# Scores of the next tile between the state's part and D, one output group per tile, D in a bank of its own

## The chip, the cores and the metric

The kernel runs on one core of a Trainium2 chip. The time is the device time of one execution in microseconds (us). The kernel before takes 898.84 us, the median of 3 runs (898.82 to 900.29).

## What is computed

Three layers follow one another. Everything is fp32, and the matmuls of the layers split each operand into a high and a low part (three products for one).

```python
# linear attention with decay, B=4 H=8 S=768 D=64
state = gamma * state + outer(k[t], v[t]);  y[t] = scale * q[t] @ state
# x: (3072, 512).  Layer 1, d_ff 1024:
h = x @ w_in;  sm = exp(h - max(h)) / (sum + 1e-9);  solu = h * sm
x = layernorm(solu) * g_ln @ w_out
# Layer 2, d_ff 2048:
h = x @ w_in;  out = (h * cos(h)) @ w_out
```

## The kernel before

The first half of the kernel (up to about 380 us) runs attention and layer 1 over 24 tiles of 128 tokens, six per batch. The second half runs layer 2 and is not touched. A tile passes through stages that are spread over several steps, so in step n the engines work on tiles n down to n - 4. One list, `STEP`, gives the stages of a step in order, each with how many tiles it lies behind. Every engine runs the same list in order and skips the names that it has no code for. Nothing but semaphores ties the engines together. The first tiles have lists of their own (`pe_first`, `act_first`, `dve_first`, `pool_first`), and a tail of hand-written order ends the half.

The stages on TensorE (PE), with the line of each matmul:

- SC (L558): scores of a tile, 16 instructions with 64 rows each, pairs of heads side by side. They fill banks 0 and 1 of PSUM (`ps_p`).
- OS (L582): the part of the output that comes from the state, 8 instructions. Left out for the first tile of a batch.
- DL (L570): D, the tile's own contribution to the state, 16 instructions with 64 columns each. It writes `ps_d`, which lies over banks 0 and 1, so SC must wait until the state has been brought up to date, and DL until the scores have been read. Left out for the last tile of a batch.
- OP (L599): masked scores times v, 16 instructions. OS and OP add up in `ps_o`, two pairs of heads in bank 2 and two in bank 3, and `o_done` rises twice per tile.
- L1a, L1b (L318 to L321, the three products): layer 1's first matrix, 12 instructions of 512 columns for each half.
- T0, T1 (L636): transposes of the centred result. T1 waits for z_l of T0, T0 for VectorE's CEN.
- L2a, L2b: layer 1's second matrix, 24 instructions. YT (L671): transposes of its result.

VectorE (DVE) masks the scores (L1055, SC), takes the low parts of x (L1076, O0 and O1) and of z (L1129, T0 and T1), takes the row maximum (L1095, L1b), copies YT (L1141), multiplies h by exp (L1101, U), adds D to the state (L1070, ST), centres (L1115, CEN), and in between splits the second layer's weights into low parts (L1149, WE, and L1144, WD). ScalarE (ACT) makes the high parts (x_h L774, z_h L800), exp (L794), the square (L809), y (L805) and the high parts of the weights (L815, L818, both in WH at the end of a step, ahead of the next step's T0). GpSimd (POOL) scales q (L967) and k, decays the state (L980) and adds weights.

SyncE (SP) issues all DMAs. `swap_unit` stores what WD and WE made and loads the next weights; it waits for WE of the last unit before it stores that unit (L457) and loads the next one (L461), which ScalarE's L818 waits for. There is one such unit in tiles 0 to 4 of the last three batches and one in the first batch.

Of the kernel before, what the change touches and what calls it, by code (L numbers as in the profile page):

```python
# [26 lines left out]
F32 = mybir.dt.float32  # L27
# [3 lines left out]
B, H, S, D = 4, 8, 768, 64  # L31
PAIRS = H // 2
# [52 lines left out]

STEP = [("PK", 0), ("PV", 0), ("SG", 1), ("L1a", 2), ("SC", 1), ("T0", 3), ("L1b", 2), ("T1", 3),
        ("EX", 2), ("OS", 1), ("DL", 1), ("OP", 1), ("YT", 4), ("U", 2), ("O0", 1), ("O1", 1), ("ST", 1),
        ("WS", 0), ("WE", 1), ("L2a", 3), ("SQ", 2), ("L2b", 3), ("CEN", 2), ("VAR", 2),
        ("WH", 0), ("WD", 0)]
LAG = 4  # L90


def build(nc, qT, kT, kn, vn, consts, w1_in, w1_out, g_ln, w2_in, w2_out, y_scratch, w2_split,
          w2o_split, out):
    ctx = ExitStack()
    with ctx:
# [5 lines left out]
        ps_p = bank[:, 0:2, :].rearrange("p a (c t) -> p c a t", c=PAIRS)  # L102
        ps_o = bank[:, 2:4, 0:2 * C]

        ps_d = bank[:, 0:2, :].rearrange("p g (j n) -> p (g j) n", j=2)[:, :, 0:D]
        ps_h = bank[:, 4:6, :]
# [133 lines left out]
        def unit(b, n):  # L240
# [8 lines left out]
                    ("L1a0", 0), ("L1b0", 0), ("L1a1", 0), ("L1b1", 0), ("SC", 2), ("OS", 2),  # L249
                    ("DL", 2), ("OP", 2), ("L1a", 1), ("T0", 0), ("L1b", 1), ("T1", 0), ("LA", 0),  # L250
                    ("LB", 0), ("LC", 0), ("LD", 0)]
        act_first = [("O0", 0), ("O1", 0), ("W1H", 0), ("W1H", 1), ("O0", 1), ("O1", 1), ("W1H", 2),
                     ("W1H", 3), ("EX", 0), ("W1H", 4), ("O0", 2), ("SQ", 0), ("O1", 2), ("W1H", 5),
                     ("T0", 0), ("W1H", 6), ("W1H", 7), ("T1", 0), ("EX", 1), ("SQ", 1), ("LD", 0)]
        dve_first = [("QS", 0), ("ID", 0), ("SC0", 0), ("SC1", 0), ("O0", 0), ("ST", 0), ("O1", 0),
# [4 lines left out]
                     ("CEN", 1), ("VAR", 1)]  # L260
# [29 lines left out]
        def wait_state(eng, s, batch, tile):  # L290

            wait(eng, s, batch, tile // TILES * (TILES - 1) + min(tile % TILES, TILES - 2),
                 per_batch=TILES - 1)
# [31 lines left out]
        def rows(a):  # L325

            return slice(a * D, (a + 1) * D)
# [56 lines left out]
        def _(sp):  # L384
# [12 lines left out]
            def load_next(t, slot):  # L397


                sp.wait_ge(o_done, 2 * t)  # L400
                if isinstance(t, int) and t == 1:
                    sp.wait_ge(d_done, 1)
                load_kq(t + 2, slot)
                load_nv(t + 2, slot)
# [118 lines left out]
            load_y(0)  # L523
            sp.wait_ge(o_done, 2 * NT)
            load_split(0, 0)
# [19 lines left out]
        def _(pe):  # L545
            def step(name, t, b):
                par = t % 2
                if name == "SC":

                    wait(pe, q_sc, b, t)  # L550
                    if t % TILES > 0:
                        wait_state(pe, st_done, b, t - 1)
                    wait(pe, pm_done, b, t - 1, 2, 1)
# [8 lines left out]
                elif name == "DL" and t % TILES < TILES - 1:  # L562

                    wait(pe, n_sc, b, t)
                    wait(pe, pm_done, b, t, 2, 1)
                    for p in range(PAIRS):
# [7 lines left out]
                elif name == "OS" and t % TILES > 0:  # L574
# [4 lines left out]
                    wait(pe, q_sc, b, t)  # L579
                    wait(pe, xl_done, b, t - 1, 2, 1)  # L580
                    for p in range(PAIRS):
                        pe.matmul(ps_o[:, p // 2, p % 2 * C:(p % 2 + 1) * C],  # L582
                                  s_32[:, (t % TILES - 1) % 2, p, :, :].rearrange("p a n -> p (a n)"),
                                  raw[:, t % RAW, 0, p * C:(p + 1) * C],
                                  start=p % 2 == 0, stop=False)
                elif name == "OP":
# [3 lines left out]
                    else:  # L590
                        wait(pe, n_sc, b, t)
                    wait(pe, xl_done, b, t - 1, 2, 1)
                    for p in range(PAIRS):
                        if p % 2 == 0:
                            wait(pe, pm_done, b, t, 2, p // 2)
                        for a in range(2):
                            h = slice((2 * p + a) * D, (2 * p + a + 1) * D)
                            o = slice((p % 2 * 2 + a) * C, (p % 2 * 2 + a + 1) * C)
                            m = pe.matmul(ps_o[rows(a), p // 2, p % 2 * C:(p % 2 + 1) * C],  # L599
                                          raw[:, t % RAW, 3, h], p_m[:, p // 2, o],  # L600
                                          start=p % 2 == 0 and t % TILES == 0, stop=p % 2 == 1,
                                          tile_position=(0, a * D))
                        if p % 2 == 1:
                            m.then_inc(o_done, 1)
                elif name[:3] in ("L1a", "L1b"):
# [5 lines left out]
                    for k in ks:  # L611
                        if half == 0 and isinstance(b, int) and t == 0:
                            pe.wait_ge(w1_lo, k + 1)
                        if half == 0 and k % 2 == 0:
                            wait(pe, xl_done, b, t, 2, k // 2)
                        m = products(pe, ps_h[:, half, :], [
                            (x_h[:, par, k, :], x_l[:, par, k, :],
                             w1i_h[:, k, cols], w1i_l[:, k, cols])], k == 0, k == KD - 1)
# [146 lines left out]
        def _(act):  # L765
# [3 lines left out]
            def step(name, t, b):  # L769
                par = t % 2  # L770
                if name in ("O0", "O1"):
                    g = int(name == "O1")
                    wait(act, o_done, b, t, 2, g)
                    act.copy(x_h[:, par, 2 * g:2 * g + 2, :],  # L774
                             ps_o[:, g, :].rearrange("p (j t) -> p j t", j=2))\
                        .then_inc(xh_done, 1)
                elif name == "W1H":
# [50 lines left out]
            def y_hi(i, p):  # L828
                if p in (P1, P2, P3):
                    act.wait_ge(ld_y, i * 16 + 16)  # L830
                else:
                    block_wait(act, {P6: t2_done, P5: t1_done, P7: t3_done, P4: t4_done}[p],
                               i, 1, 0)
                if isinstance(i, int) and i == 0:
                    act.wait_ge(o_done, 2 * NT)
                else:
                    at(act, p_done[p], i, -1)
                act.copy(yc_h[:, p, :, :], operand[p]).then_inc(yh_done, 1)
# [119 lines left out]
        def _(pool):  # L958
            pool.memset(mhalf[:, :], -0.5).then_inc(setup, 1)

            def step(name, t, b):
# [12 lines left out]
                elif name == "SG" and 0 < t % TILES < TILES - 1:  # L974
                    c = t % TILES
                    wait_state(pool, st_done, b, t - 1)
                    wait(pool, o_done, b, t - 1, 2, 1)
                    new, old = [s_32[:, n % 2, :, :, :].rearrange("p c a n -> p c (a n)")
# [55 lines left out]
        def _(dve):  # L1034
# [4 lines left out]
            def step(name, t, b):  # L1039
# [5 lines left out]
                elif name == "QS":  # L1045
                    q = raw[:, t % RAW, 0, :]
                    loaded(dve, ld_kq, t, b)
                    dve.tensor_tensor(q, q, qsc, ALU.mult).then_inc(q_sc, 1)
                elif name in ("SC", "SC0", "SC1"):
                    if isinstance(b, int) and t == 0:  # L1050
                        dve.wait_ge(ld_mask, 16)
                    for g in [int(name[2])] if name[2:] else range(2):
                        wait(dve, qk_done, b, t)
                        wait(dve, o_done, b, t - 1, 2, g)
                        dve.tensor_tensor(two_pairs(p_m[:, g, :]), ps_p[:, 2 * g:2 * g + 2, :, :],  # L1055
                                          mask[:, 4 * g:4 * g + 4, :].rearrange(
                                              "p (j a) t -> p j a t", j=2),
                                          ALU.mult).then_inc(pm_done, 1)
                elif name == "ST" and c < TILES - 1:

                    wait_state(dve, d_done, b, t)
                    wait(dve, o_done, b, t - 1, 2, 1)
                    new = s_32[:, c % 2, :, :, :]
# [8 lines left out]
                    m.then_inc(st_done, 1)  # L1072
                elif name in ("O0", "O1"):
                    g = int(name == "O1")
                    wait(dve, xh_done, b, t, 2, g)
                    dve.tensor_tensor(x_l[:, par, 2 * g:2 * g + 2, :],  # L1076
                                      ps_o[:, g, :].rearrange("p (j t) -> p j t", j=2),
                                      x_h[:, par, 2 * g:2 * g + 2, :].bitcast(F32),
                                      ALU.subtract).then_inc(xl_done, 1)
# [261 lines left out]
```

## Time and profile before

| | |
|---|---|
| median of 3 runs | 898.84 us |
| profiled execution | 900.71 us |
| its span (first to last instruction) | 898.9 us |
| TensorE busy | 883.4 us (98%) |
| VectorE busy | 570.6 us (63%) |
| ScalarE busy | 439.3 us (49%) |
| GpSimd busy | 142.5 us (16%) |
| granted TensorE clock, mean | 1.000 |

A busy TensorE counts overlapping matmuls once. The pitch, from one instruction's start to the next one's, tells what an instruction costs. A matmul of 512 columns has a duration of 0.39 us and a pitch of 0.23 us.

### The profile page before, as it was taken

The numbers are of one execution on the slowest core, as the hardware profiler recorded it, in microseconds if no ns is written. First come the engines' busy times: TensorE is split into PE (matmuls) and PEld (weight loads), VectorE is DVE, ScalarE is ACT, GpSimd is POOL, SyncE is SP. The second block draws the span as 40 slices with busy tenths as digits, with TensorE's granted clock in tenths as the row PEclk, the third lists the DMA queues.
The fourth block names the chain that finished last, engine by engine and source line by source line (L and its number), as shares of the span: only waits on it lengthen the run. The fifth ranks groups of instructions, "written<-read, shape, count | busy, mean of one in ns | idle before, by whom it ended". The sixth has DMA issues, their size and how long they took to land.

```text
span 898.9 us, 14463 instructions
## 1 busy us (share of the span) xinstructions
PE 883.4 (98%) x5184; PEld 771.0 (86%) x5184; DVE 570.6 (63%) x872; ACT 439.3 (49%) x687; POOL 142.5 (16%) x187
## 2 busy tenths in 40 slices
PE   5899999999999999999999999999999999999998
PEld 4788888888888888889999999899999999999997
DVE  4956566566665666576665866566765658765654
ACT  3433344244333434366555755455655547554553
POOL 3242434225333342310000000000000000000000
PEclk9999999999999999999999999999999999999999
DMA  9534465636555463758954447444365444454401
GB/s 340 177 113 131 158 223 171 215 111 233 205 177 174 166 241 118 235 187 300 305 190 118 120 115 249 134 112 123 110 198 186 120 115 118 119 183 121 113 0 71
DMA packets 106662, 148.18 MB, mean 165 GB/s; under 512 B 7424, under 2 KB 77184, under 8 KB 106624
## 3 DMA queue, kind: packets, MB, share of 16 engines
q1 hardware_dynamic: 106624, 147.69, 51.3%
q8 instruction: 21, 0.34, 0.2%
q14 instruction: 17, 0.14, 0.0%
HBM read 112.01 MB, written 35.65 MB: 164 GB/s over the span
## 4 chain that ended last, share of the span: by engine, by line
PE 96%; DVE 2%; DMA 1%; issue 1%; SPq 0%; ACT 0%; DVEq 0%
PE bank L318 28%; PE bank L321 28%; PE bank L320 28%; PE bank L558 3%; PE bank L636 3%; PE bank L599 2%; PE bank L582 2%; PE bank L671 2%; PE bank L570 1%; DVE w1i_l L1084 1%; DMA raw<-kT 1%; DVE w1o_l L1089 0%; DVE nmax L1095 0%; DMA out<-o_a 0%; DVE s L1070 0%
## 5 line engine op out<-in xcount | busy, mean ns | idle before, releaser
L318 PE MATMUL bank<-yc_h,ring 128*128 128x384 f32 x448 | 151.5, 338 | 0.0
L320 PE MATMUL bank<-yc_l,ring 128*128 128x384 f32 x448 | 151.4, 338 | 0.0
L321 PE MATMUL bank<-yc_h,ring 128*128 128x384 f32 x448 | 150.9, 337 | 0.0
L1178 DVE SCALAR_TENSOR_TENSOR gg<-turns,c 128x768 f32<-128x768 int32 x64 | 61.0, 954 | 63.8 <-ACT turns L846 63.8
L852 ACT ACTIVATE gg<-gg 128x768 f32<-128x768 f32 x64 | 54.1, 846 | 80.2 <-DVE gg L1185 80.1
L846 ACT ACTIVATE turns<-c 128x768 int32<-128x768 f32 x64 | 54.2, 846 | 79.1 <-DVE c L1248 76.6
L318 PEld LDWEIGHTS bank<-yc_h,ring 128*128 128x128 f32 x448 | 84.1, 188 | 8.0 <-issue 0.5
L320 PEld LDWEIGHTS bank<-yc_l,ring 128*128 128x128 f32 x448 | 84.2, 188 | 7.2
L321 PEld LDWEIGHTS bank<-yc_h,ring 128*128 128x128 f32 x448 | 84.1, 188 | 0.0
L318 PE MATMUL bank<-w1i_h,x_h 128*128 128x512 f32 x192 | 77.5, 404 | 1.6 <-DVE w1i_l L1084 1.6
L318 PE MATMUL bank<-w1o_h,z_h 128*128 128x512 f32 x192 | 77.2, 402 | 1.1 <-DVE z_l L1129 1.1
L321 PE MATMUL bank<-w1o_h,z_l 128*128 128x512 f32 x192 | 75.2, 391 | 0.0
L321 PE MATMUL bank<-w1i_h,x_l 128*128 128x512 f32 x192 | 75.0, 391 | 0.0
L321 PE MATMUL bank<-w2o,glo_l 128*128 128x512 f32 x192 | 75.0, 391 | 0.0
L320 PE MATMUL bank<-w2o,glo_h 128*128 128x512 f32 x192 | 75.0, 391 | 0.0
L320 PE MATMUL bank<-w2o,ghi_h 128*128 128x512 f32 x192 | 74.9, 390 | 0.0
L800 ACT CAST z_h<-bank 128x512 fp32r<-128x512 f32 x48 | 28.2, 587 | 95.5 <-PE bank L636 95.5
L320 PE MATMUL bank<-w1i_l,x_h 128*128 128x512 f32 x192 | 74.8, 390 | 0.0
L321 PE MATMUL bank<-w2o,ghi_l 128*128 128x512 f32 x192 | 74.8, 390 | 0.0
L320 PE MATMUL bank<-w1o_l,z_h 128*128 128x512 f32 x192 | 74.7, 389 | 0.0
L318 PE MATMUL bank<-w2o,glo_h 128*128 128x512 f32 x192 | 74.6, 389 | 0.0
L318 PE MATMUL bank<-w2o,ghi_h 128*128 128x512 f32 x192 | 74.6, 388 | 0.0
(99 smaller groups left out, 1701.3 us busy)
## 6 DMA issues: line engine op xcount, KB each, us to landing
ring<-w_split SPq DMA_DIRECT2D x224, 256.0 KB, 2.8
w_split<-w_out SPq DMA_DIRECT2D x16, 896.0 KB, 6.3
w2o_split<-wo_out SPq DMA_DIRECT2D x16, 512.0 KB, 2.9
w2o<-w2o_split SPq DMA_DIRECT2D x8, 1024.0 KB, 7.7
raw<-qT SPq DMA_DIRECT2D x24, 256.0 KB, 4.4
raw<-kT SPq DMA_DIRECT2D x24, 256.0 KB, 3.5
raw<-kn SPq DMA_DIRECT2D x24, 256.0 KB, 4.5
raw<-vn SPq DMA_DIRECT2D x24, 256.0 KB, 5.1
```

Of the source, the lines that this page charges most:

```text
L318: eng.matmul(dst, ah, bh, start=first and i == 0, stop=False, skip_group_check=read_between)
L320: eng.matmul(dst, ah, bl, start=False, stop=False, skip_group_check=read_between)
L321: m = eng.matmul(dst, al, bh, start=False, stop=last_one and i == n - 1, skip_group_check=read_between)
L558: m = pe.matmul(ps_p[:, p, a, :], raw[rows(a), t % RAW, 1, cols], raw[rows(a), t % RAW, 0, cols], start=True, stop=True, tile_position=(a ...
L582: pe.matmul(ps_o[:, p // 2, p % 2 * C:(p % 2 + 1) * C], s_32[:, (t % TILES - 1) % 2, p, :, :].rearrange("p a n -> p (a n)"), raw[:, t % RA ...
L599: m = pe.matmul(ps_o[rows(a), p // 2, p % 2 * C:(p % 2 + 1) * C], raw[:, t % RAW, 3, h], p_m[:, p // 2, o], start=p % 2 == 0 and t % TILES ...
L636: m = pe.transpose(ps_t[:, k * 128:(k + 1) * 128], c_b[:, (4 * g + k) * 128:(4 * g + k + 1) * 128], ident[:, :])
L671: m = pe.transpose(ps_t[:, k * 128:(k + 1) * 128], y32[:, k * 128:(k + 1) * 128], ident[:, :])
L800: act.copy(z_h[:, 4 * g:4 * g + 4, :].rearrange("p k t -> p (k t)"), ps_t[:, :])\
L846: act.activation(turns[:, r, :], flat(c_32[:, r, :, :]), ACT.Copy, scale=INV_2PI)\
L852: act.activation(gg[:, r, :], gg[:, r, :], ACT.Sin, scale=0.5)\
L1178: dve.scalar_tensor_tensor(gg[:, r, :], turns[:, r, :], -TWO_PI_HI, flat(c_32[:, r, :, :]), ALU.mult, ALU.add)\
```

## The change

SC of tile n moves from its place after L1a of step n + 1 (where it was one tile behind) to step n, between OS and DL of tile n - 1. The masking on VectorE gets the name SM and stands between U and X. Output and D get one bank each (2 and 3), apart from the scores. The output is one accumulation group per tile: the first pair alone starts it, `o_done` rises once, and O0 and O1 become one operation X on ScalarE and one on VectorE. SC no longer waits for the state; DL waits for the previous state in place of p_m. L1a waits for all of x_l at once. In the opening SC of tile 3 comes before the first L2 products, and in the tail there is no SC left.

```diff
-STEP = [("PK", 0), ("PV", 0), ("SG", 1), ("L1a", 2), ("SC", 1), ("T0", 3), ("L1b", 2), ("T1", 3),
-        ("EX", 2), ("OS", 1), ("DL", 1), ("OP", 1), ("YT", 4), ("U", 2), ("O0", 1), ("O1", 1), ("ST", 1),
-        ("WS", 0), ("WE", 1), ("L2a", 3), ("SQ", 2), ("L2b", 3), ("CEN", 2), ("VAR", 2),
-        ("WH", 0), ("WD", 0)]
+STEP = [("PK", 0), ("PV", 0), ("SG", 1), ("L1a", 2), ("T0", 3), ("L1b", 2), ("T1", 3), ("EX", 2),
+        ("OS", 1), ("SC", 0), ("DL", 1), ("OP", 1), ("YT", 4), ("U", 2), ("SM", 0), ("X", 1),
+        ("ST", 1), ("WS", 0), ("WE", 1), ("L2a", 3), ("SQ", 2), ("L2b", 3), ("CEN", 2),
+        ("VAR", 2), ("WH", 0), ("WD", 0)]
...
-        ps_o = bank[:, 2:4, 0:2 * C]
-        ps_d = bank[:, 0:2, :].rearrange("p g (j n) -> p (g j) n", j=2)[:, :, 0:D]
+        ps_o = bank[:, 2, :].rearrange("p (c t) -> p c t", c=PAIRS)
+        ps_d = bank[:, 3, 0:PAIRS * D].rearrange("p (c n) -> p c n", c=PAIRS)
...
         pe_first = [("SC", 0), ("OP", 0), ("DL", 0), ("SC", 1), ("OS", 1), ("DL", 1), ("OP", 1),
                     ("L1a0", 0), ("L1b0", 0), ("L1a1", 0), ("L1b1", 0), ("SC", 2), ("OS", 2),
-                    ("DL", 2), ("OP", 2), ("L1a", 1), ("T0", 0), ("L1b", 1), ("T1", 0), ("LA", 0),
-                    ("LB", 0), ("LC", 0), ("LD", 0)]
+                    ("DL", 2), ("OP", 2), ("L1a", 1), ("T0", 0), ("L1b", 1), ("T1", 0), ("SC", 3),
+                    ("LA", 0), ("LB", 0), ("LC", 0), ("LD", 0)]
...
                 if name == "SC":
                     wait(pe, q_sc, b, t)
-                    if t % TILES > 0:
-                        wait_state(pe, st_done, b, t - 1)
                     wait(pe, pm_done, b, t - 1, 2, 1)
...
                 elif name == "DL" and t % TILES < TILES - 1:
                     wait(pe, n_sc, b, t)
-                    wait(pe, pm_done, b, t, 2, 1)
+                    wait_state(pe, st_done, b, t - 1)
...
-                            m = pe.matmul(ps_o[rows(a), p // 2, p % 2 * C:(p % 2 + 1) * C],
+                            m = pe.matmul(ps_o[rows(a), p, :],
                                           raw[:, t % RAW, 3, h], p_m[:, p // 2, o],
-                                          start=p % 2 == 0 and t % TILES == 0, stop=p % 2 == 1,
+                                          start=p == 0 and t % TILES == 0, stop=p == PAIRS - 1,
                                           tile_position=(0, a * D))
-                        if p % 2 == 1:
-                            m.then_inc(o_done, 1)
+                    m.then_inc(o_done, 1)
...
-                if name in ("O0", "O1"):
-                    g = int(name == "O1")
-                    wait(act, o_done, b, t, 2, g)
-                    act.copy(x_h[:, par, 2 * g:2 * g + 2, :],
-                             ps_o[:, g, :].rearrange("p (j t) -> p j t", j=2))\
-                        .then_inc(xh_done, 1)
+                if name == "X":
+                    wait(act, o_done, b, t)
+                    act.copy(x_h[:, par, :, :], ps_o).then_inc(xh_done, 1)
...
-                elif name in ("SC", "SC0", "SC1"):
+                elif name in ("SM", "SC0", "SC1"):
...
-                elif name in ("O0", "O1"):
-                    g = int(name == "O1")
-                    wait(dve, xh_done, b, t, 2, g)
-                    dve.tensor_tensor(x_l[:, par, 2 * g:2 * g + 2, :],
-                                      ps_o[:, g, :].rearrange("p (j t) -> p j t", j=2),
-                                      x_h[:, par, 2 * g:2 * g + 2, :].bitcast(F32),
+                elif name == "X":
+                    wait(dve, xh_done, b, t)
+                    dve.tensor_tensor(x_l[:, par, :, :], ps_o, x_h[:, par, :, :].bitcast(F32),
                                       ALU.subtract).then_inc(xl_done, 1)
```

## Rows read from the trace of the kernel before

**Rows 1.** The page's first part: busy time, share and instructions of each engine.
```profile
PE 883.4 (98%) x5184; PEld 771.0 (86%) x5184; DVE 570.6 (63%) x872; ACT 439.3 (49%) x687; POOL 142.5 (16%) x187
```

**Rows 2.** TensorE's waits: line, releaser, us in total, times, longest.
```profile
PE bank L318 <- DVE w1i_l L1084: 1.6, 2, 1.0
PE bank L318 <- DVE z_l L1129: 1.1, 1, 1.1
PE bank L558 <- issue: 1.0, 1, 1.0
...
PE bank L570 <- DVE p_m L1055: 0.4, 1, 0.4
```

**Rows 3.** TensorE in order of time, one step: start, duration, operation, count.
```profile
204.98 0.39 PE L321 MATMUL bank<-w1i_h,x_l 128*128 128x512 f32 x1
205.30 1.16 PE L558 MATMUL bank<-raw 64*128 64x128 f32 x16
206.39 0.66 PE L636 MATMUL bank<-ident,work 128*128 128x128 f32 x4
206.81 0.48 PE L318 MATMUL bank<-w1i_h,x_h 128*128 128x512 f32 x1
...
209.65 0.60 PE L636 MATMUL bank<-ident,work 128*128 128x128 f32 x4
210.08 1.06 PE L582 MATMUL bank<-raw,s 128*128 128x128 f32 x8
211.07 0.69 PE L570 MATMUL bank<-raw 128*64 128x64 f32 x16
...
225.70 0.60 PE L636 MATMUL bank<-ident,work 128*128 128x128 f32 x4
```

**Rows 4.** The same view in the opening, around T0 of tile 0.
```profile
33.86 0.39 PE L321 MATMUL bank<-w1i_h,x_l 128*128 128x512 f32 x1
...
34.45 0.48 PE L318 MATMUL bank<-w1i_h,x_h 128*128 128x512 f32 x1
```

**Rows 5.** VectorE in order of time, the same step.
```profile
206.51 1.29 DVE L1055 TENSOR_TENSOR p_m<-bank,cst 128x512 f32<-128x512 f32 x2 [0.81 <-PE bank L558]
207.72 0.68 DVE L1129 TENSOR_TENSOR z_l<-bank,z_h 128x512 fp32r<-128x512 f32 x1
...
213.35 0.69 DVE L1141 COPY work<-bank 128x512 f32<-128x512 f32 x1 [1.68 <-PE bank L671]
213.96 1.22 DVE L1101 SCALAR_TENSOR_TENSOR work<-bank,work 128x1024 f32<-128x1024 f32 x1
...
215.38 0.76 DVE L1076 TENSOR_TENSOR x_l<-bank,x_h 128x256 fp32r<-128x256 f32 x2
216.05 0.84 DVE L1070 TENSOR_TENSOR s<-s,bank 64x256 f32<-64x256 f32 x2
216.92 0.69 DVE L1149 TENSOR_TENSOR wo_out<-wo_raw,wo_out 128x512 fp32r<-128x512 f32 x1
```

**Rows 6.** SyncE's issues of the weight load, two of the twelve.
```profile
107.14 0.38 SPq L461 DMA_DIRECT2D wo_raw<-w_out  x1
...
218.20 0.38 SPq L461 DMA_DIRECT2D wo_raw<-w_out  x1
```

**Rows 7.** ScalarE's copies of these loads, in brackets its idle time before.
```profile
112.37 0.62 ACT L818 CAST wo_out<-wo_raw 128x512 fp32r<-128x512 f32 x1 [3.18 <-DMA wo_raw<-w_out]
...
221.79 0.62 ACT L818 CAST wo_out<-wo_raw 128x512 fp32r<-128x512 f32 x1 [1.53 <-DMA wo_raw<-w_out]
```

**Rows 8.** VectorE's z_l, in the opening and behind the slow load.
```profile
40.92 0.67 DVE L1129 TENSOR_TENSOR z_l<-bank,z_h 128x512 fp32r<-128x512 f32 x1
...
113.52 0.69 DVE L1129 TENSOR_TENSOR z_l<-bank,z_h 128x512 fp32r<-128x512 f32 x1 [0.73 <-ACT z_h L800]
```

**Rows 9.** TensorE's matmul that waited for the first of these.
```profile
41.74 0.47 PE L318 MATMUL bank<-w1o_h,z_h 128*128 128x512 f32 x1 [1.07 <-DVE z_l L1129]
```

**Rows 10.** The loads of wo_raw, all 16: us from issue to landing.
```profile
DMA to landing us min/median/max: 3.2/3.5/5.9
```

More of the change, by code:

```diff
@@ L249, in build @@
                     ("L1a0", 0), ("L1b0", 0), ("L1a1", 0), ("L1b1", 0), ("SC", 2), ("OS", 2),
-                    ("DL", 2), ("OP", 2), ("L1a", 1), ("T0", 0), ("L1b", 1), ("T1", 0), ("LA", 0),
-                    ("LB", 0), ("LC", 0), ("LD", 0)]
[L252 to L255, printed above, removed]
[4 rows of a table removed]
[2 rows of a table added]
+        act_first = [("X", 0), ("W1H", 0), ("W1H", 1), ("X", 1), ("W1H", 2), ("W1H", 3), ("EX", 0),
+                     ("W1H", 4), ("X", 2), ("SQ", 0), ("W1H", 5), ("T0", 0), ("W1H", 6), ("W1H", 7),
+                     ("T1", 0), ("EX", 1), ("SQ", 1), ("LD", 0)]
+        dve_first = [("QS", 0), ("ID", 0), ("SC0", 0), ("SC1", 0), ("X", 0), ("ST", 0), ("SC0", 1),
[4 rows of a table added]
                      ("CEN", 1), ("VAR", 1)]
@@ L397, in load_next @@
             def load_next(t, slot):
-                sp.wait_ge(o_done, 2 * t)
+                sp.wait_ge(o_done, t)
                 if isinstance(t, int) and t == 1:
@@ L523, in _ @@
             load_y(0)
-            sp.wait_ge(o_done, 2 * NT)
+            sp.wait_ge(o_done, NT)
             load_split(0, 0)
@@ L579, in step @@
                     wait(pe, q_sc, b, t)
-                    wait(pe, xl_done, b, t - 1, 2, 1)
+                    wait(pe, xl_done, b, t - 1)
                     for p in range(PAIRS):
-                        pe.matmul(ps_o[:, p // 2, p % 2 * C:(p % 2 + 1) * C],
+                        pe.matmul(ps_o[:, p, :],
                                   s_32[:, (t % TILES - 1) % 2, p, :, :].rearrange("p a n -> p (a n)"),
                                   raw[:, t % RAW, 0, p * C:(p + 1) * C],
-                                  start=p % 2 == 0, stop=False)
+                                  start=p == 0, stop=False)
                 elif name == "OP":
@@ L591, in step @@
                         wait(pe, n_sc, b, t)
-                    wait(pe, xl_done, b, t - 1, 2, 1)
+                    wait(pe, xl_done, b, t - 1)
                     for p in range(PAIRS):
@@ L613, in step @@
                             pe.wait_ge(w1_lo, k + 1)
-                        if half == 0 and k % 2 == 0:
-                            wait(pe, xl_done, b, t, 2, k // 2)
+                        if half == 0 and k == 0:
+                            wait(pe, xl_done, b, t)
                         m = products(pe, ps_h[:, half, :], [
@@ L834, in y_hi @@
                 if isinstance(i, int) and i == 0:
-                    act.wait_ge(o_done, 2 * NT)
+                    act.wait_ge(o_done, NT)
                 else:
@@ L976, in step @@
                     wait_state(pool, st_done, b, t - 1)
-                    wait(pool, o_done, b, t - 1, 2, 1)
+                    wait(pool, o_done, b, t - 1)
                     new, old = [s_32[:, n % 2, :, :, :].rearrange("p c a n -> p c (a n)")
@@ L1048, in step @@
                     dve.tensor_tensor(q, q, qsc, ALU.mult).then_inc(q_sc, 1)
-                elif name in ("SC", "SC0", "SC1"):
+                elif name in ("SM", "SC0", "SC1"):
                     if isinstance(b, int) and t == 0:
                         dve.wait_ge(ld_mask, 16)
-                    for g in [int(name[2])] if name[2:] else range(2):
+                    for g in range(2) if name == "SM" else [int(name[2])]:
                         wait(dve, qk_done, b, t)
-                        wait(dve, o_done, b, t - 1, 2, g)
+                        wait(dve, o_done, b, t - 1)
                         dve.tensor_tensor(two_pairs(p_m[:, g, :]), ps_p[:, 2 * g:2 * g + 2, :, :],
@@ L1061, in step @@
                     wait_state(dve, d_done, b, t)
-                    wait(dve, o_done, b, t - 1, 2, 1)
+                    wait(dve, o_done, b, t - 1)
                     new = s_32[:, c % 2, :, :, :]
```

8 rows, old and new, of the table dve_first are left out of this document.

## The prediction

> **What bounds the kernel now.** I read the page's shares first, then who waited for whom on TensorE, then TensorE's own order of time in one step of the first half, and last the same step on the other engines. TensorE is busy 98% of the span [rows 1], and its waits are few and nearly all in the opening: 1.6 us for the low parts of the first weights, 1.1 us for z_l, 1.0 us at the second score group, 0.4 us for p_m [rows 2]. From step 4 to the end of the first half it never waits, so the length of a step is the sum of its instructions' pitches: T1 starts at 209.65 and at 225.70, 16.05 us [rows 3]. The step is shorter where tile 0 of a batch has no OS or tile 5 no DL, by the same amount before and after. So a change in this half is worth what it takes out of TensorE's own order, as long as nothing else comes to need more than 16 us per step. The other engines have no such reserve without limit, and that is where I look below. The second half is not touched.
>
> **Part 1, the move of SC on TensorE.** In the old place (after L1a, before T0) the time from the last L1a matmul to the first of L1b is 206.81 - 204.98 = 1.83 us [rows 3]. The opening has the same boundary without SC: 34.45 - 33.86 = 0.59 us [rows 4]. Taking SC out saves 1.24 us. In the new place it stands between OS and DL. It takes 206.39 - 205.30 = 1.09 us from its first instruction to the next group's first, and OS takes 211.07 - 210.08 = 0.99 us with the step to another shape in it [rows 3]. OS to SC and SC to DL are not in this trace. If a 64-row group hands over to a 64-column group for nothing, SC costs about 1.00 (1.09 less the 0.09 us by which it started late behind L1a: 205.30 - 204.98 = 0.32 against the usual 0.23). If the entry costs a gap of its own beyond the one in OS's 0.99, and another 0.08 is lost, it costs 1.26. I take 1.09, the row nearest to it, so a step saves 1.24 - 1.09 = 0.15 us, bounds -0.02 and 0.24. TensorE's own need is then 15.90 us.
>
> What the row shows is that the first SC instruction starts 0.32 us behind the last full matmul where 0.23 is usual [rows 3]. The Trainium skill, "TensorEngine Tiling (Array Packing)", Key Properties, says that changing the tiling mode drains TensorE, whichever two modes it is. The old order changes mode four times in a step (full, 64 rows, full, 64 columns, full), the new one three times. By the rule the saving is there and no hand-over is free. By the 0.32 row alone the saving could also be lost at SC to DL. The rule is one more reason for a value inside my bounds and no term of the sum.
>
> The move is made in 20 steps (4 to 23). A 21st SC leaves the tail, and the SC of tile 3 goes to the end of the opening. The tail gains the full 1.24 us. OS, DL, OP and YT keep their counts. Grouping the output in one bank (start on the first pair alone, one completion instead of two) removes no matmul. I cost it at 0.
>
> **Part 2, ACT and VectorE.** O0 and O1 become one X: VectorE's two halves take 216.05 - 215.38 = 0.67 us, one operation of 512 columns 0.61 by z_l's row of that shape (its pitch to the next row). ScalarE saves a little too. Both have spare time there and TensorE waits for neither. Value 0, and 24 fewer instructions on each. L1a now waits for the whole of x_l, and DL for the previous state and no longer for p_m. Both are ready more than a microsecond before.
>
> **Part 3, what the order does to VectorE's queue.** The masking of the scores used to run in an idle stretch before T0 (206.51, two operations, next start 207.72: 1.21 us [rows 5]). It now stands behind U and ahead of X, ST, WE, CEN and VAR. YT's copy leads that queue and waits for TensorE's YT, which comes 1.09 us later after T1 than before, because SC now lies between. Count from T1's start (209.65). Before: copy at 3.70 (213.35), U at 4.31 (213.96), O0 at 5.73 (215.38), ST at 6.40 (216.05), WE at 7.27 (216.92) [rows 3, 5]. After: copy at 4.79, U at 5.40, masking at 6.82, X at 8.03, ST at 8.64, WE at 9.51. WE is 2.24 us later relative to T1.
>
> Who waits for WE? It is the low part of a second-layer weight. SyncE stores that weight behind it and then issues the load of the next one, 1.28 us after WE's start (218.20 - 216.92) [rows 5, 6]. ScalarE's queue holds the copy of that load (L818) ahead of the next step's T0 copy, whose z_l in turn is what TensorE's T1 waits for. Call D the time from the issue to the start of L818: 3.59 us here, 5.23 in the slow case [rows 6, 7]. From L818 to the start of z_l's subtraction is 113.52 - 112.37 = 1.15 us [rows 7, 8], and from there to TensorE 41.74 - 40.92 = 0.82 us [rows 9]. The loop from T1 to T1 is thus 9.51 + 1.28 + D + 1.97 = 12.76 + D. Before it was 10.52 + D, at most 15.75 us, and hidden. After, TensorE's own 15.90 us is reached at D = 3.14. There are 12 such steps (four in each of the last three batches). In all twelve ScalarE waited for the load. Their D sum to 43.0, the median is 3.36, the first and slowest 5.23. The load's own time to landing is 3.2 us at best, 3.5 median, 5.9 worst [rows 10]. So the late wait is T1 on z_l, L2 and all that is behind it on TensorE moves along, and each of these steps costs 12.76 + D - 16.05 = D - 3.29 us against before. By the median that is 0.07 each, 0.8 in all. By this trace's sum it is 43.0 - 39.5 = 3.5 us, of which 1.9 come from the one slow load. I take 2.0: a slow load in some runs, not in all. The step without OS has 0.83 less on both sides and the same difference.
>
> SyncE's other DMAs (four loads of q, k and v, the y store, the w_split store, the w_raw load) also move about 2 us later in the step. They are used a step or more later. ScalarE's wait for w_raw's sums has about 3 us left. The longer VectorE queue also delays GpSimd's scaling of q for the next SC, which still ends nearly 4 us ahead of it.
>
> **Part 4, the opening.** SC of tile 1 no longer waits for the state, so the 1.0 us wait shrinks. The masking, and the W1 low parts behind it, start about 1 us earlier, and with them both waits of the 1.6 us. DL no longer waits 0.4 us on p_m, but L1a of tile 1 then waits on U. At its end SC of tile 3 (1.09) comes in, partly in the 1.1 us wait for z_l, and its masking (1.21) pushes the last W1 low part. Together between -1.5 and +0.4 us, and I take -0.6. The move leaves no more to gain there, since VectorE sets that stretch.
>
> **Sum.** 8 steps x -0.15 = -1.2. 12 steps +2.0. Tail -1.24. Opening -0.6. Together -1.0 us. The profiled execution's own time is 900.71 us (span 898.9 and 1.8 around it), so 899.7. The median of the runs shown is 898.84, 1.87 below the profiled one (the profile itself seems to cost that), and -1.0 on it gives 897.8 us. The times of the rivals below stand on the median too.
>
> **The rivals.**
> A, no loop. If VectorE's queue is shorter than counted or the load lands sooner by 0.25 us, T1 never waits, and all 20 steps keep 0.15: -3.0 - 1.24 - 0.6 = -4.8, 894.0 us. For it: the loop passes TensorE's need by only 0.22 us at the median. Against it: every term is a row of this trace, and in one step the old order already started z_l only 0.3 us before it would have cost time (113.52 + 0.82 = 114.34, T1 was due at 114.64).
> B, the wait takes more than the move gives, and the kernel is slower. Place: T1, behind ScalarE's L818. Price: D - 3.29 in 12 steps. With -1.2 - 1.24 - 0.6 = -3.0 on the other side it decides from a mean D of 3.54, and it is slower by over 1.8 us from 3.69. At 3.83 it is 6.5 - 3.0 = +3.4, 902.3 us. For it: the mean here is 3.58, and the store of 0.5 MB just ahead with 1 MB of loads just behind share the queues. Against: ten of the twelve were under 3.6.
> C, SC is as dear between OS and DL as before (0 saved per step): 12 steps +2.0 (TensorE's own need 16.05, the loop 16.12 or more), tail -1.24, opening -0.6: +0.2, 899.0 us.
>
> **How the numbers follow.** About 0.2% (1.8 us) is what a measurement can tell from no change. The forecast has 0.45, A 0.25, B 0.2, C 0.1. Within the forecast's own range of -3 to +1 (895.8 to 899.8) a quarter lies beyond -1.8. Faster: 0.25 + 0.12 = 0.37. Slower: B less its mild end, 0.18. The same: 0.45. The 8-in-10 range goes from half a microsecond inside A to near B: 894.5 to 902.0.
>
> **What would show it.** In the profile after: SC's 16 instructions between OS and DL, with 1.0 to 1.2 us to DL's first. L1a's last to L1b's first 0.59 us. T1 to T1 15.9 us in the steps without such a load. In the 12 others WE at about T1 + 9.5, L818 waiting for the load, and a new row among TensorE's waits, z_l, 12 times, some 0.2 us each. The forecast is wrong if that row is missing (A), if it sums to more than 6 us (B), or if the steps without it are still 16.05 (C).

## The result and the profile after

The changed kernel takes 906.0 us (median of 4 runs, 903.0 to 907.0) against 899.6 for the kernel before (4 runs). The ratio is 1.0061, 95% interval 1.0042 to 1.0080: slower by about 0.6%. I had forecast 897.8 us, no change or a little less, with 894.5 to 902.0 as the range. The profiled execution after took 903.04 us (span 901.2), the shortest of the four.

The page's first part, columns as before: TensorE is busy for 1.9 us less than in [rows 1] while the span is longer, so it waits more.

```profile
PE 881.5 (98%) x5184; PEld 770.1 (85%) x5184; DVE 566.1 (63%) x848; ACT 436.1 (48%) x663; POOL 143.7 (16%) x187
```

TensorE's waits after, to set beside [rows 2]: a new first row, T1 (L633 now) on VectorE's z_l. It has 6 waits and not 12, and its 6.8 us pass the 6 us that the prediction had named as the sign of rival B.

```profile
PE bank L633 <- DVE z_l L1120: 6.8, 6, 1.4
PE bank L556 <- DVE raw L1042: 6.2, 1, 6.2
PE bank L318 <- DVE w1i_l L1075: 1.2, 1, 1.2
...
PE bank L318 <- DVE w1o_l L1080: 0.7, 1, 0.7
```

TensorE in order of time after, a step in the second full batch, to set beside [rows 3]. T0 stands directly between L1a and L1b now (0.35 us from its start to L1b's, as in the opening before), and SC between OS and DL takes 213.56 - 212.46 = 1.10 us.

```profile
207.66 0.60 PE L633 MATMUL bank<-ident,work 128*128 128x128 f32 x4
208.01 0.48 PE L318 MATMUL bank<-w1i_h,x_h 128*128 128x512 f32 x1
...
210.98 0.66 PE L633 MATMUL bank<-ident,work 128*128 128x128 f32 x4
211.48 1.06 PE L580 MATMUL bank<-raw,s 128*128 128x128 f32 x8
212.46 1.16 PE L556 MATMUL bank<-raw 64*128 64x128 f32 x16
213.56 0.69 PE L568 MATMUL bank<-raw 128*64 128x64 f32 x16
```

The loop, in the first full batch (batch 1). First T1 (the view ends inside it and shows 3 of its 4 instructions), then VectorE's queue behind it (to set beside [rows 5]), SyncE's load and ScalarE's copy [rows 6, 7], z_l [rows 8] and the next T1.

```profile
111.85 0.55 PE L633 MATMUL bank<-ident,work 128*128 128x128 f32 x3 [1.41 <-DVE z_l L1120]
```
```profile
116.70 0.69 DVE L1132 COPY work<-bank 128x512 f32<-128x512 f32 x1 [2.85 <-PE bank L668]
117.31 1.22 DVE L1092 SCALAR_TENSOR_TENSOR work<-bank,work 128x1024 f32<-128x1024 f32 x1
...
118.80 1.29 DVE L1049 TENSOR_TENSOR p_m<-bank,cst 128x512 f32<-128x512 f32 x2
120.00 0.68 DVE L1069 TENSOR_TENSOR x_l<-bank,x_h 128x512 fp32r<-128x512 f32 x1
120.60 0.84 DVE L1064 TENSOR_TENSOR s<-s,bank 64x256 f32<-64x256 f32 x2
121.47 0.69 DVE L1140 TENSOR_TENSOR wo_out<-wo_raw,wo_out 128x512 fp32r<-128x512 f32 x1
```
```profile
122.76 0.38 SPq L461 DMA_DIRECT2D wo_raw<-w_out  x1
```
```profile
127.50 0.62 ACT L812 CAST wo_out<-wo_raw 128x512 fp32r<-128x512 f32 x1 [3.89 <-DMA wo_raw<-w_out]
128.03 0.58 ACT L794 CAST z_h<-bank 128x512 fp32r<-128x512 f32 x1
```
```profile
128.64 0.69 DVE L1120 TENSOR_TENSOR z_l<-bank,z_h 128x512 fp32r<-128x512 f32 x1 [3.90 <-ACT z_h L794]
```
```profile
129.38 0.66 PE L633 MATMUL bank<-ident,work 128*128 128x128 f32 x4 [1.39 <-DVE z_l L1120]
```

Read it from T1 to T1. WE starts 9.62 us behind T1 (predicted 9.51), the load is issued at 10.91, ScalarE's copy of it starts D = 4.74 us later, and the next T1 another 1.88 us later. That is 17.53 us. The predicted loop, 12.76 + D, gives 17.50. In [rows 3] the step was 16.05.

Where the time went, by T1's starts in the two traces: T1 of tile 0 comes 3.70 us earlier (33.61 against 37.31), of which 0.9 us is that the first load landed earlier. How much of the rest is the change's varies: T1 of tile 0 starts at 36.3 to 37.3 us in the three traces of the old order (two of them from experiments below) and at 33.2 to 35.5 in the nine with SC in its new place. The step after it gives 0.06. The eight steps without a load of this kind give 0.90 us in all (0.07 to 0.14 each). The twelve with one cost 6.98 us. The sum, +2.3 us, is the difference of the spans. D was 4.75, 4.74, 4.71 and 4.83 us in the first full batch, 3.31, 3.84, 3.46, 3.38 in the second and 3.95, 3.37, 3.38, 3.47 in the third, a mean of 3.93. The row of the load's time to landing has moved from [rows 10]:

```profile
DMA to landing us min/median/max: 2.8/3.9/5.6
```

### The profile page after: what moved, and what is told of

Same layout as the page of the kernel before. It is cut to its first block, busy times and chain, and to the rows that moved or that the text cites. A ratio compares the mean times of both kernels' runs of the same rounds, so it can differ in the third digit from the quotient of the medians.

```text
span 901.2 us, 14411 instructions
## 1 busy us (share of the span) xinstructions
PE 881.5 (98%) x5184; PEld 770.1 (85%) x5184; DVE 566.1 (63%) x848; ACT 436.1 (48%) x663; POOL 143.7 (16%) x187
## 4 chain that ended last, share of the span: by engine, by line
PE 86%; DVE 6%; DMA 4%; issue 2%; ACT 1%; SPq 0%; DVEq 0%; ACTq 0%
PE bank L321 25%; PE bank L318 25%; PE bank L320 25%; DMA wo_raw<-w_out 3%; PE bank L556 3%; PE bank L597 2%; PE bank L633 2%; PE bank L580 2%; PE bank L668 2%; PE bank L568 1%; DVE work L1092 1%; DVE p_m L1049 1%; DVE z_l L1120 1%; DVE s L1064 1%; DVE w1o_l L1080 1%
## 5 line engine op out<-in xcount | busy, mean ns | idle before, releaser
L1182 DVE SCALAR_TENSOR_TENSOR gg<-gg,c 128x768 f32<-128x768 f32 x64 | 61.1, 955 | 13.5 <-ACT gg L852 13.5
## 6 DMA issues: line engine op xcount, KB each, us to landing
w_split<-w_out SPq DMA_DIRECT2D x16, 896.0 KB, 6.6
```

What stands on the lines that cost most here:

```text
L1182: dve.scalar_tensor_tensor(gg[:, r, :], gg[:, r, :], 0.5, flat(c_32[:, r, :, :]), ALU.subtract, ALU.mult).then_inc(g_done[r], 1)
```

## The experiments

Each ran in 5 rounds beside the kernel before (900.5 to 900.7 us in these rounds). My theory by now was the forecast's rival B, the loop through the weight load. The rival theory was that the new place of SC or of the masking costs TensorE time by itself.

### The changed kernel once more

No edit. 

> The changed kernel once more, for a second trace of how long the weight load takes. Theory (the loop): TensorE's T1 comes 12.8 us plus D after the last T1 in the 12 steps with such a load, D being the time from the issue of the load to the start of ScalarE's copy of it. In the first trace D was 4.7 us in all four steps of one batch (T1 to T1 17.5) and 3.3 to 3.9 in the others (16.0 to 16.6). The first trace was the fastest of four executions (903.0 against 905.7 to 907.0), so here I expect a second batch with D near 4.7: 905 to 907 us, and T1 to T1 = 12.8 + D in every such step. Rival (something outside the loop costs the time, such as the new place of SC itself): slow executions without longer T1 to T1 in those twelve steps.

Measured: 905.6 us (903.2 to 906.4), ratio 1.0059 (1.0045 to 1.0073). Its traced execution took 904.05, with one batch near 4.7 and not two. D was 4.75, 4.78, 5.09, 4.82 in the first full batch and 3.2 to 4.0 in the others. The four steps took 16.60, 17.57, 17.87 and 17.52 us. T1 to T1 was 12.7 to 12.8 + D in three of them and 11.85 + D in the first, which has no OS. The slower executions left no trace, so how they divide is not shown.

### WE early

```diff
-        ("OP", 1), ("YT", 4), ... ("ST", 1), ("WS", 0), ("WE", 1), ("L2a", 3), ...
+        ("OP", 1), ("WE", 1), ("YT", 4), ... ("ST", 1), ("WS", 0), ("L2a", 3), ...
```

> The changed kernel with WE (the low part of the second layer's weight) moved on VectorE from behind ST to ahead of YT, into its idle stretch after T1; nothing else is changed. Loop theory: WE starts near T1 + 2.1 instead of T1 + 9.6, so the load is issued over 7 us earlier and ScalarE never holds T0 back; all steps fall to TensorE's own 15.9 us, and the wait of TensorE on z_l is gone. From the first trace (903.0, of which 8.6 us lie above 15.92 per step in the 12 steps): 894.3 us, about 0.6% faster than before, with little spread. Rival (the later masking or the new place of SC costs TensorE time by itself): stays within 2 us of the changed kernel, 903 to 907.

Measured: 895.9 us (895.5 to 896.1), ratio 0.9954 (0.9941 to 0.9967), 1.6 us above what I expected and 7 below the rival. One name moved in VectorE's list takes 10 us off the changed kernel. WE starts 1.94 us behind T1, the load is issued at 3.2, and it lands 3.2 to 3.4 us later in the first full batch too. TensorE, in the step and batch that took 17.5 us above:

```profile
127.95 0.60 PE L633 MATMUL bank<-ident,work 128*128 128x128 f32 x4
...
143.87 0.60 PE L633 MATMUL bank<-ident,work 128*128 128x128 f32 x4
```

15.92 us, and so in every full step (one with OS and DL). Its waits have no row on z_l:

```profile
PE bank L556 <- DVE raw L1042: 7.2, 1, 7.2
PE bank L318 <- DVE w1i_l L1075: 1.0, 1, 1.0
PE bank L597 <- DVE p_m L1049: 1.0, 1, 1.0
PE bank L318 <- DVE w1o_l L1080: 0.7, 1, 0.7
PE bank L318 <- DVE work L1092: 0.2, 1, 0.2
```

### The copy behind T0

```diff
-        ... ("L1a", 2), ("T0", 3), ("L1b", 2), ...
+        ... ("L1a", 2), ("T0", 3), ("WO", 1), ("L1b", 2), ...
...
                     act.copy(w_out[:, :, 0, :], w_raw[:, A11:, :]).then_inc(wi_hi, 1)
+                elif name == "WO" and unit(b, t) is not None:
+                    u = unit(b, t)
                     unit_wait(act, ld_wo, b, u, 16)
```

> The changed kernel with ScalarE's copy of the weight load (second half of WH) moved behind T0 of the next step. The load is issued as late as before and may land as late; only what is queued behind it changes. Loop theory (what costs is ScalarE's queue, the copy ahead of z_h of T0): T0's z_h is never late, 894.3 us as with WE early, D still 3.3 to 4.7 in the trace. Rival (the late load costs through the weight chain itself, WE and SyncE behind it, or through its traffic): 900 us or more, TensorE waiting elsewhere.

Measured: 896.1 us (894.7 to 897.4), ratio 0.9955 (0.9941 to 0.9968). This is the sharper of the two cures. The load is issued as late as in the changed kernel (10.85 us behind T1) and still takes long. ScalarE still waits for it, but T0 is no longer queued behind. SyncE, ScalarE and TensorE:

```profile
123.05 0.38 SPq L461 DMA_DIRECT2D wo_raw<-w_out  x1
```
```profile
127.80 0.62 ACT L814 CAST wo_out<-wo_raw 128x512 fp32r<-128x512 f32 x1 [1.66 <-DMA wo_raw<-w_out]
```
```profile
128.12 0.60 PE L633 MATMUL bank<-ident,work 128*128 128x128 f32 x4
...
144.04 0.60 PE L633 MATMUL bank<-ident,work 128*128 128x128 f32 x4
```

D is 4.75 us and T1 to T1 15.92. What costs is not the late load but what stands behind its copy on ScalarE.

### The load ahead of the store

```diff
+                if new is not None:
+                    ... sp.dma_start(wo_raw, w2_out of the next unit)
                 if old is not None:
                     ... sp.dma_start(w2o_split, wo_out)
-                if new is not None:
-                    ... sp.dma_start(wo_raw, w2_out of the next unit)
```

> The changed kernel with SyncE issuing the load of the next weight (0.25 MB) ahead of the store of the last one (0.5 MB) instead of behind it. The load is issued 0.43 us earlier, so the loop is 12.35 + D. Theory that the store in front is what makes D: D falls to 2.9 to 3.2 in all steps, the loop ends below 15.9 and the kernel takes 894 to 895 us. Rival (D is set by the loads and stores behind it, or by a phase of the queues): the 4.7 us stay in some batches, 17.05 us per step there, about 4 us per slow batch above 894.5: 896 to 904.

Measured: 907.5 us (905.9 to 912.3), ratio 1.0081 (1.0067 to 1.0095), so neither. The load itself did what the first theory said, 2.8 to 3.1 us in all twelve steps. But D rose to between 4.1 and 6.2, and ScalarE's waits tell why:

```profile
ACT wo_out L812 <- DMA w2o_split<-wo_out: 40.2, 12, 4.8
```

ScalarE's copy writes into the buffer that the store still reads, so it also waits for the store, the larger of the two, which was now second. I had not counted this second wait. In the shipped order the store lands 2.9 to 3.6 us after its issue and is always ahead of the load. The first full batch is slow here too, but now for the store: it landed 4.2 to 5.6 us after its issue there and 3.5 to 4.0 in the others. So it is the second of the two transfers that is slow in that batch, whichever it is. As long as both use this buffer, turning their order doesn't help.

The trace shows a second cost. T1's two longest waits, 2.32 and 2.21 us, were each followed by a granted TensorE clock of 0.50, its lower level (1.2 GHz): from 114.6 to 116.0 and from 169.0 to 171.0 us. OS took 1.91 us there in place of 1.06. In the changed kernel T1's longest wait was 1.4 us, 1.7 in its second trace, and the clock stayed at 1.00 behind them.

### The masking back

```diff
-        ... ("L1a", 2), ("T0", 3), ... ("U", 2), ("SM", 0), ("X", 1), ...
+        ... ("L1a", 2), ("SM", 1), ("T0", 3), ... ("U", 2), ("X", 1), ...
...
-                     ("L1b", 1), ("T1", 0), ("SC0", 3), ("SC1", 3), ("W1L", 7), ("U", 1),
+                     ("L1b", 1), ("T1", 0), ("W1L", 7), ("U", 1),
```

> The changed kernel with the masking of the scores (SM) back in VectorE's old idle place, ahead of T0's z_l of the next step; SC stays between OS and DL. The late masking's 1.21 us leave the queue ahead of WE, so WE starts at T1 + 8.4 and the loop is 11.6 + D. Loop theory: with D of 3.3 it stays under TensorE's 15.9, with the 4.7 of the first full batch it passes it by 0.3 to 0.4 us, four times: 1.5 us above the kernel with WE early (895.9), less 0.7 us because the masking of tile 3 no longer holds up the last W1 low part in the opening: 896 to 897 us. Rival (the later YT copy, by 1.1 us, is enough to keep the wait): 902 us or more.

Measured: 896.0 us (894.3 to 896.5), ratio 0.9952 (0.9939 to 0.9965). WE starts at 8.2 to 8.3 behind T1, and little but the slow loads (D 4.74, 4.96, 4.96) stretches its step, to 15.28 (15.03 otherwise), 16.43 and 16.44 us. T1's waits on z_l are 0.6 us in all:

```profile
PE bank L633 <- DVE z_l L1120: 0.6, 2, 0.3
```

So 1.2 us of VectorE's queue were most of the loss, the later YT copy alone the smaller part.

### The banks and X alone

```diff
-        ... ("L1a", 2), ("T0", 3), ... ("OS", 1), ("SC", 0), ("DL", 1), ... ("SM", 0), ("X", 1), ...
+        ... ("L1a", 2), ("SC", 1), ("SM", 1), ("T0", 3), ... ("OS", 1), ("DL", 1), ... ("X", 1), ...
...
-  ... ("T1", 0), ("SC", 3),   (TensorE's opening)   ... ("SC0", 3), ("SC1", 3),   (VectorE's)
+  ... ("T1", 0),                                    ...
```

> The changed kernel with SC and the masking both back in their old places in the step, and no SC of tile 3 in the opening; what is left of the change is the banks, the single output group, X as one operation, and the waits that go with them. TensorE's step is 16.05 us again, no wait on z_l (loop 10.5 + D). What is left is the gain of the opening. My estimate for it was -0.6 us; the two traces show that T1 of tile 0 comes 3.7 us earlier, 0.9 of it because the first load landed earlier. Theory: 899.6 less 2.5 to 3.5, so 896 to 898 us, and SC's move is worth about 3 us (20 steps of 0.13 to 0.15) against the kernels without the wait, 895.9. Rival (the opening's gain is luck of the first loads): 899 to 900.5.

Measured: 898.7 us (897.0 to 900.7, 12 runs), ratio 0.9981 (0.9972 to 0.9989). The step is 16.05 us again. The gain, 1.8 us, is clear of noise but below the 2.5 to 3.5 that I expected, so some of the 3.7 us by which T1 of tile 0 came earlier in the first trace was not this part's. Where the gain sits is not shown: the traced execution is the slowest of the twelve, with a granted TensorE clock of 0.59 from 24 to 26 us and 0.56 from 26 to 28 us. Against WE early (895.9) the median leaves 2.8 us for SC's move, as 20 steps of 0.14 would give.

### WE late in the kernel before

```diff
-        ("WS", 0), ("WE", 1), ("L2a", 3), ("SQ", 2), ("L2b", 3), ("CEN", 2), ("VAR", 2),
+        ("WS", 0), ("L2a", 3), ("SQ", 2), ("L2b", 3), ("CEN", 2), ("VAR", 2), ("WE", 1),
...
                         .then_inc(cen_done, 1)
+                    for k in range(0 if isinstance(b, int) else 2):
+                        dve.tensor_scalar(w1_raw[:, 5 + (2 * t + k) % 3, :], u_b,
+                                          nmu[:, par:par + 1], None, ALU.add)
```

> The kernel before, its SC, banks and masking untouched, with WE moved on VectorE behind VAR and with two more operations of CEN's kind (1.3 us, into space that nothing reads) from batch 1 on, so that WE starts near T1 + 9.7 as it does in the changed kernel (9.6). Loop theory: it costs what it costs there, 12.95 + D against TensorE's own 16.05 in 12 steps: at D of 3.4 in eight and 4.7 in four steps 2.4 + 6.4 = 9 us above before, 907 to 911 us, with TensorE waiting for z_l. Rival (the new place of SC is needed for the loss): within 2 us of before.

Measured: 904.4 us (903.4 to 906.6), ratio 1.0050 (1.0036 to 1.0065). The loss is there with SC, the masking and the banks untouched. It is 3.8 us and not 9, and its twelve steps take 3.8 us more than in the trace before. Only one load took long (D 4.85), and the other eleven stayed at 3.2 to 3.5. WE started 9.6 to 10.1 us behind T1 in the full steps. In the slow step it was 10.11, and the step took 148.07 - 129.96 = 18.11 us:

```profile
129.96 0.66 PE L636 MATMUL bank<-ident,work 128*128 128x128 f32 x4
...
148.07 0.66 PE L636 MATMUL bank<-ident,work 128*128 128x128 f32 x4 [1.85 <-DVE z_l L1132]
```

### WE early in the kernel before

The same move as in the first cure, made in the old order. 

> The kernel before with WE ahead of YT on VectorE and nothing else changed. Loop theory: in the old order the loop (10.5 + D) is below TensorE's own 16.05 already, so there is nothing to gain: 899.5 to 900.7 us, the same as before, and T1 to T1 at 16.05 in every step. Rival (WE early is a gain by itself, whatever SC does): 895 to 897 us, and the gain of the changed kernel with WE early is not SC's.

Measured: 900.1 us (898.7 to 901.0, 12 runs), ratio 0.9995 (0.9986 to 1.0004). No change, and 16.05 us per step. The 10 us that this move brings in the changed kernel are the loop's alone.

### The loads of q, k and v ahead

```diff
-                swap_unit(b, n)          # w_split, w_raw, w2o_split, wo_raw
-                load_next(t, (n + 2) % RAW)
+                swap_w1(b, n)            # w_split, w_raw
+                load_next(t, (n + 2) % RAW)
+                swap_w2(b, n)            # w2o_split, wo_raw
                 store_yt(t - LAG)
```

> The changed kernel with SyncE issuing the four loads of q, k and v ahead of its wait for WE instead of right behind the weight load. Store and load of the weight keep their order and their issue time (T1 + 10.9), but 1 MB of loads behind them is gone and only the y store follows. Theory that the 4.7 us come from the traffic behind the load: it lands in 3.2 to 3.4 us in all batches, the loop is 12.8 + 3.3 = 16.1, 0.2 us above own need: 897 to 899 us. Rival (the store in front, or the place in memory): the 4.7 us stay in the first full batch, 904 to 906 us.

Measured: 907.8 us (903.8 to 913.6), ratio 1.0095 (1.0069 to 1.0122). The load takes 5.0 to 5.2 us in the first full batch and 3.4 to 3.6 in the others: the 1 MB behind it is not what makes it slow. The rival holds in that batch. In the others D is 3.51 us on average, against 3.52 in the first trace of the changed kernel. The traced execution is the fastest of the six. The slowest three had a mean granted clock of 0.994 to 0.998, so a part of their time may be TensorE's clock, as in the kernel with the load ahead of the store. They left no trace that would show it.

### Another place in memory

In the kernel with the copy behind T0, every full batch loads batch 2's units (`pick(w2_out, turned, new)` with `turned` at 2) and leaves out its own. 

> The changed kernel with the copy behind T0 (no wait on TensorE there), where every full batch loads the second-layer output weights of batch 2's units again instead of its own, so the output's last layer has wrong weights; all the work is done. It asks why the load takes 4.7 us in the first full batch and 3.3 in the others. If the place in memory that it is read from sets it, D is 3.2 to 3.8 in all batches now. If not (the store's place, or the order of traffic in that batch), the 4.7 to 4.9 us stay in the first full batch. The time is no test: 896 us either way.

Measured: 896.9 us (896.5 to 897.2). D is 4.81, 5.86, 4.92, 4.88 in the first full batch and 3.2 to 3.6 in the others. The place that is read is not the cause.

### Both cures

```diff
+        ("L1a", 2), ("SM", 1), ("T0", 3), ... ("OP", 1), ("WE", 1), ("YT", 4), ("U", 2), ("X", 1), ...
```

> The changed kernel with both cures: WE ahead of YT, and the masking back ahead of T0's z_l. The loop is gone and the opening keeps its 1.1 us (with the masking back T1 of tile 0 to T1 of tile 1 took 13.3 us in place of 14.4). From 896.0 with the masking back, less the 1.3 us that its trace shows in four steps above 15.92: 894.7 us, the fastest of these kernels. Rival: the two do not add, 895.9.

Measured: 894.6 us (894.4 to 895.0), ratio 0.9938 (0.9925 to 0.9950). This is the fastest version, 6.0 us below the kernel before and about 11 below the changed one. All full steps take 15.92 us, and T1 of tile 0 to T1 of tile 1 is 13.34 us in place of 14.36.

## Why the prediction was wrong

The step that failed is the term "12 steps +2.0", that is, D: the steps cost 7.0 and 6.7 us in the two traces of the changed kernel. I had the place, the chain and its length: 12.76 + D against 12.79 + D measured. I took D between the median (3.36) and the mean (3.58) of the old trace, and treated the one slow load (5.23) as chance, "a slow load in some runs, not in all". Both traces of the changed kernel have it four times in a row, in the first full batch, with a mean over the twelve steps of 3.93 and 3.91. It was no chance in the old order either: the traces of the kernel before, of the banks alone and of WE late in the kernel before have it once each, always in that batch. The medians (905.6 and 895.9 without the loop) put the whole cost of the loop at about 10 us. So the forecast's own rival B came true, at a price beyond the range. Its point of decision, a mean D of 3.54, was passed. It had a chance of 0.2 from me when the old trace's own mean of 3.58 was already past that point. Taking less than the trace showed was a choice for which no row spoke.

The sum also stood on a start that was too low. I read the 1.87 us between the profiled execution and the median as the cost of the profile. In the rounds of the experiments the kernel before takes 900.5 to 900.7 us in the median (898.5 to 901.5), and both profiled executions of the changed kernel are among the faster ones of theirs. So no run shows such a cost, and 898.84 was a low draw. It doesn't save the forecast: 906.0 lies outside the range from either start.

Point by point:

- SC's move: 0.15 us per step was predicted, from 16.05 to 15.90. Measured 15.92, and SC takes 1.10 us in its new place (predicted 1.09). A free hand-over from 64 rows to 64 columns would have given 1.00, one that costs a gap of its own 1.26, so one change of mode less per step is worth 0.13 us.
- Rival A, no loop: -4.8 us was its price. The kernel with WE early gives 895.9 - 900.7 = -4.8. The sum of everything but the loop was right, in part by luck: SC's move gave 2.6 us (3.0 predicted), opening and tail 2.2 (1.8 predicted), and the two misses cancel.
- Opening and tail: -1.8 us was predicted for both. In the version without the loop it is -4.8 + 20 x 0.13 = -2.2. The banks alone, which leave the tail as it was, measured -1.8 us. How much belongs to the opening and how much to the tail is not shown.
- VectorE's queue: copy at 4.79, masking at 6.82, WE at 9.51 was predicted, and 4.85, 6.95, 9.62 stand in the trace.
- Rival C, no gain from the move: excluded by the 15.92.
- ACT's and VectorE's saved instructions at 0: nothing in the traces speaks against it. It wasn't tried alone.
- Not seen by me: ScalarE's copy waits for the store as well as for the load. It did not matter in the shipped order, but it decided one experiment against my expectation.

What stays open is why the second of the two transfers is slow in the first full batch (the load mostly 4.7 us and more, against 3.3 in the others). The traffic issued behind it and the place it is read from are excluded. The place that the store writes to was not tried. The traces hold a candidate that I didn't test. The profile lists two small DMA queues that it calls "instruction". Q8 moved 21 packets of about 16 KB in the whole changed kernel. In the first full batch, the first pass of the loop over batches, it moves about one in each step, and none from 195 to 260 us, in the second pass. Twelve traces have the store right ahead of the load, with 12 such loads each, and 26 of these 144 loads took 4.7 us or more. A q8 packet fell between issue and landing in all 26, 2.2 to 3.1 us after the issue in 25 of them and 3.8 in one. Three more loads had a q8 packet 3.0 to 3.5 us after the issue and landed in 3.2 to 3.3. The 115 loads without one landed in 3.2 to 4.1. In the three traces with WE early no q8 packet falls between issue and landing, and all their loads landed in 3.2 to 4.1. This would also explain why the slow loads keep to one batch. But it is a coincidence in time and no more: no run moved these packets, and how one of 16 KB would hold a load back by 1.4 us is not shown.

How the executions of the changed kernel without a trace lose another 2 to 4 us is open too. Their mean granted clock is 0.999 or 1.000, so TensorE's clock accounts for 1 us at most.

## What to carry to other kernels

An operation moved into a helper engine's queue delays all that stands behind it there. Follow the last of these, through the DMA that it triggers, to the engine whose queue waits for that DMA, and add up the whole loop from one step to the next. If the loop comes near the step (here within 0.2 us by the median), price it with the slowest landings of the trace and not the median, and look whether the longest of them keep to one place in the program: a wait that used to be hidden shows its spread as soon as it is not. The cures are cheap and of two kinds: do the work that starts the DMA in an idle stretch ahead of the queue, or put the copy that waits for it behind what the critical engine needs.

## What the runs showed of the hardware

- A load of 256 KB issued about 0.43 us behind a store of 512 KB landed in 3.2 to 4.1 us in 118 of 144 cases (12 steps in each of 12 traces) and in 4.7 to 5.8 us in 26, all in the first full batch. Issued ahead of the store it landed in 2.8 to 3.1 us each time, and the store behind it took 4.2 to 5.6 us in that batch and 3.5 to 4.0 in the others.
- All 26 slow loads had a packet of the profile's instruction queue q8 between issue and landing. Of the 118 others 3 had one before 3.6 us, about when they landed. That one causes the other is not shown.
- The slow batch has three or four slow loads in the kernels that issue the load 9.5 to 11 us behind T1 in the full steps of the new order (the changed one twice traced, the copy behind T0, the masking back, the loads ahead, the other place), with TensorE waiting or not. It has one in the kernel before, in the banks alone and in WE late in the kernel before, the last of which issues it as late as the changed kernel (10.7 to 11.4 us behind T1 in the full steps). So the distance from T1 alone does not decide it.
- In the kernel with the load ahead of the store, waits of TensorE of 2.32 and 2.21 us were followed by a granted clock of 0.50 (1.2 GHz). T1's waits of up to 1.7 us in the changed kernel were not.
- TensorE needs about 1.1 us for 16 fp32 instructions of 64 rows and 128 columns, whether full-array products or ones of 64 columns come next to them.
